# The fifth key tiles of two attention heads as one tile, with mask rows, and the last queries' part added on VectorE

## The reference

```python
scores = scale * np.matmul(q, k.transpose(0, 1, 3, 2))
mask = block_i >= block_j                 # blocks of 64
scores = np.where(mask, scores, -1000000000.0)
scores = scores - np.max(scores, axis=-1, keepdims=True)
attn = np.exp(scores)
attn = attn / (np.sum(attn, axis=-1, keepdims=True) + 1e-09)
return np.matmul(attn, v).astype(np.float32)
```

## Time and profile before

| | |
|---|---|
| median of 3 runs | 1044.92 us (1044.06 to 1045.32) |
| profiled execution | 1045.19 us, its span 1043.0 us |
| mean granted TensorE clock | 0.991 |
| PE busy | 1014.5 us, 97% |
| PE weight loads busy | 933.6 us, 90% |
| POOL busy | 533.9 us, 51% |
| VectorE busy | 443.0 us, 42% |
| ScalarE busy | 368.3 us, 35% |
| DMA, mean | 120 GB/s |

### The profile page before, as it was taken

The page is one execution under the profiler, slowest core; times in us unless marked ns, Lnnn a source line. Parts: engine busy times, 40 slices in busy tenths (PEclk is TensorE's granted clock), DMA queues, the critical chain, the costliest instruction groups (busy, mean ns, idle before and its releaser), DMA issues.

```text
span 1043.0 us, 16716 instructions
## 1 busy us (share of the span) xinstructions
PE 1014.5 (97%) x5927; PEld 933.6 (90%) x5928; DVE 443.0 (42%) x935; ACT 368.3 (35%) x681; POOL 533.9 (51%) x424
## 2 busy tenths in 40 slices
PE   6999999898999999999999999999999999999996
PEld 5899999787989898989899998889898989899895
DVE  6788888674224233332425652222232223222221
ACT  5999988843212222222224413212121212111110
POOL 8689999530000202020202136968778887878752
PEclk9999999999999999999999999999999999999998
DMA  8787886292970101010301166262717163634303
GB/s 174 165 199 193 208 209 169 73 282 75 367 298 2 61 0 61 0 61 0 127 15 62 52 222 177 79 180 69 193 32 217 23 191 70 191 71 141 41 8 45
DMA packets 73682, 125.27 MB, mean 120 GB/s; under 512 B 13073, under 2 KB 30609, under 8 KB 73634
## 3 DMA queue, kind: packets, MB, share of 16 engines
q1 hardware_dynamic: 64594, 103.74, 33.8%
q0 software_dynamic: 8960, 20.61, 9.9%
q10 hardware_dynamic: 80, 0.29, 0.1%
HBM read 78.73 MB, written 36.67 MB: 111 GB/s over the span
## 4 chain that ended last, share of the span: by engine, by line
PE 74%; DVE 1%; ACT 0%; POOLq 0%; issue 0%; DVEq 0%
PE ps_turn L1639 13%; PE ps_x L1615 10%; PE ps_b L1615 10%; PE ps_a L1686 10%; PE ps_x L1704 9%; PE ps_b L1686 9%; PE ps_small L1639 8%; PE ps_a L1595 2%; PE ps_small L1587 1%; PE ps_turn L1577 1%; PE ps_small L1569 0%; POOLq L894 0%; PE ps_small L1570 0%; DVE y_tile L1380 0%; DVE w_raw L1545 0%
## 5 line engine op out<-in xcount | busy, mean ns | idle before, releaser
L1142 POOL DMA_INDIRECT expert_rows<-x_rows,slot_idx x36 | 41.7, 1158 | 307.6 <-DVE slot_idx L1515 298.5
L1199 POOL DMA_INDIRECT out<-y_tile,out_rows x40 | 63.3, 1581 | 76.1 <-DVE y_tile L1380 71.5
L1242 ACT CAST xT_high<-ps_a 128x512 fp32r<-128x512 f32 x40 | 23.3, 587 | 190.3 <-PE ps_a L1595 190.3
L1317 ACT COPY prod<-ps_a 128x384 f32<-128x384 f32 x48 | 23.0, 480 | 163.7 <-PE ps_b L1686 163.7
L1522 DVE TENSOR_TENSOR prod<-ps_b,prod 128x384 f32<-128x384 f32 x48 | 26.8, 557 | 125.5 <-ACT prod L1317 125.5
L1615 PE MATMUL ps_b<-xT_high,w_high 128*128 128x256 f32 (+3 forms) x256 | 77.5, 303 | 0.0
L1639 PE MATMUL ps_turn<-wo_high,hT_high 128*128 128x512 f32 x192 | 76.2, 397 | 1.2 <-DVE hT_low L1371 1.2
L1615 PE MATMUL ps_x<-xT_high,w_high 128*128 128x256 f32 (+3 forms) x256 | 76.9, 300 | 0.0
L1615 PE MATMUL ps_x<-xT_low,w_high 128*128 128x256 f32 (+3 forms) x256 | 76.8, 300 | 0.0
L1615 PE MATMUL ps_x<-xT_high,w_low 128*128 128x256 f32 (+3 forms) x256 | 76.8, 300 | 0.0
L1615 PE MATMUL ps_b<-xT_high,w_low 128*128 128x256 f32 (+3 forms) x256 | 76.8, 300 | 0.0
(11 more groups left out here) (271 smaller groups left out, 3011.7 us busy)
## 6 DMA issues: line engine op xcount, KB each, us to landing
spare<-e_w SPq DMA_DIRECT2D x16, 1024.0 KB, 5.3
w_raw<-e_w SPq DMA_DIRECT2D x16, 1024.0 KB, 8.8
expert_rows<-zeros SPq DMA_DIRECT2D x8, 1290.0 KB, 15.3
ex_rows<-expert_rows SPq DMA_DIRECT2D x40, 258.0 KB, 4.1
k_raw<-kT SPq DMA_DIRECT2D x31, 288.0 KB, 4.9
out<-zeros SPq DMA_DIRECT2D x11, 512.0 KB, 10.3
q_raw<-qT SPq DMA_DIRECT2D x16, 288.0 KB, 4.5
q_mix<-q_top SPq DMA_DIRECT2D x16, 288.0 KB, 3.8
```

The lines of the kernel that those rows point to most:

```text
L1142: nc.gpsimd.indirect_dma_start(out=rows_dram, out_offset=bass.IndirectOffsetOnAxis(ap=slot_idx[:, k, t:t + 1], axis=0), in_=x_rows[:, t, : ...
L1199: nc.gpsimd.indirect_dma_start(out=out, out_offset=bass.IndirectOffsetOnAxis(ap=out_rows[:, j:j + 1], axis=0), in_=y_tile[j][:], in_offset ...
L1242: nc.scalar.copy(xT_high[:, :, j * P:(j + 1) * P], ps_xT[j % XS][:].rearrange("p (c t) -> p c t", t=P)).then_inc(xhigh, 1)
L1317: nc.scalar.copy(prod[f % 2][:], ps_a[f % 2][:, 0:G]).then_inc(a_copied, 1)
```

## The change

The keys of both heads are put in one row of 1152: 576 of head 0, then the last 64 of head 1 (its keys are rolled by 64 on the host), then the first 512 of head 1. Columns 512 to 640 are then the fifth tiles of both heads, 64 keys each. They are one key tile for the last 64 queries of both heads, 128 in all. The cross terms (keys of one head, queries of the other) get -1e9 by two more mask rows. The zero padding of the keys goes, with its memsets.

The fifth tile moves from the units "early0" and "early1" to the unit "first", which now has 384 columns in place of 256, while the early units have 448 in place of 512. Its scores are two matmuls of 128 columns in place of four of 64, its values three of 128 in place of six of 64. v's fifth tile holds head 0's last 64 keys on partitions 0 to 63 and head 1's on 64 to 127, with ones in the other half; it is loaded by two DMAs in place of one, and cast (ACT) and subtracted (POOL) by an instruction of its own. Its output goes to its own 128 columns of heads_out, last_out, and DVE adds it to the outputs taken out, with two instructions behind its take_out and a wait between; out_whole counts them, and the gathering of sums and PE's next "first" values wait for it. ACT copies the last queries' maxima before the exps of "late1" in place of after them, and PE's "first" scores wait for both copies.

```diff
-        k_again = [sb(f"k_again{u}", [P, 2, PADDED], F32R) for u in range(OPERANDS)]
+        k_again = [sb(f"k_again{u}", [P, 2, S], F32R) for u in range(OPERANDS)]
+        last_out = heads_out[:, 512 + P:512 + P + 2 * BLOCK]
...
+        def keys_of(h, begin, end):
+            at = h * (S + BLOCK)
+            return slice(at + begin, at + end)
...
             def load_v(n):
...
                 sp.dma_start(flat[:, 0:FULL], v[n, 0:FULL * P].rearrange("(c p) e -> p c e", p=P)).then_inc(v_loaded, 16)
-                sp.dma_start(flat[0:S - FULL * P, FULL], v[n, FULL * P:S]).then_inc(v_loaded, 16)
+                for h in range(2):
+                    own = slice(h * D, (h + 1) * D)
+                    sp.dma_start(v_raw[own, FULL, h], v[n, FULL * P:S, own]).then_inc(v_loaded, 16)
...
             def gather_sums(n):
+                sp.wait_ge(out_whole, 2 * (n + 1))
                 for h in range(2):
-                    sp.wait_ge(out_taken[h], n + 1)
...
             def low_v(n):
...
                 for h in range(2):
                     part = slice(h * D, (h + 1) * D)
-                    nc.gpsimd.tensor_tensor(v_low[u][:, :, h, part], v_raw[:, :, h], v_high[u][:, :, h, part].bitcast(F32),
+                    nc.gpsimd.tensor_tensor(v_low[u][:, 0:FULL, h, part], v_raw[:, 0:FULL, h], v_high[u][:, 0:FULL, h, part].bitcast(F32),
                                             ALU.subtract).then_inc(v_low_ready, 1)
+                nc.gpsimd.tensor_tensor(v_low[u][:, FULL, 0], v_raw[:, FULL].rearrange("p h e -> p (h e)"), v_high[u][:, FULL, 0].bitcast(F32),
+                                        ALU.subtract).then_inc(v_low_ready, 1)
...
                 nc.vector.tensor_scalar(tmp[n % SLOTS][1], whole_out[1], guard[:, 1:2], None, ALU.add).then_inc(out_taken[1], 1)
+                dve.wait_ge(out_taken[1], n + 1)
+                for h in range(2):
+                    ours = tmp[n % SLOTS][h][:, LAST_AT[h]:LAST_AT[h] + BLOCK]
+                    nc.vector.tensor_tensor(ours, last_out[:, h * BLOCK:(h + 1) * BLOCK], ours, ALU.add).then_inc(out_whole, 1)
...
-                nc.scalar.copy(parts, v_raw[:]).then_inc(v_high_ready, 1)
+                nc.scalar.copy(parts, v_raw[:, 0:FULL]).then_inc(v_high_ready, 1)
+                nc.scalar.copy(v_high[u][:, FULL, 0], v_raw[:, FULL].rearrange("p h e -> p (h e)")).then_inc(v_high_ready, 1)
...
                 each(copy_max, p + 1, 0)
+                each(copy_max, p + 1, 1)
                 each(exps, p, "late1")
-                each(copy_max, p + 1, 1)
...
-                    pe.wait_ge(max_copied, 2 * n + 1)
-                    tiles = [(work[:, SHARED, h * P:(h + 1) * P], h, 0, 0, P) for h in range(2)]
+                    pe.wait_ge(max_copied, 2 * n + 2)
+                    tiles = [(work[:, SHARED, h * P:(h + 1) * P], h, keys_of(h, 0, P), slice(0, P)) for h in range(2)]
+                    tiles += [(work[:, SHARED, 2 * P:2 * P + 2 * BLOCK], slice(0, 2), slice(FULL * P, FULL * P + P), slice(S - BLOCK, S))]
...
-                    tiles = {"early": [(out[:, 0:LATER], h, 0, P, S), (out[:, LATER:LATER + BLOCK], h, 4, S - BLOCK, S)],
+                    tiles = {"early": [(out[:, 0:LATER], h, keys_of(h, 0, P), slice(P, S))],
...
+                    if n:
+                        pe.wait_ge(out_whole, 2 * n)
...
+                    for k, (vs, ps) in enumerate(parts):
+                        mm = nc.tensor.matmul(last_out, vs[:, FULL, 0], ps[:, AT_LAST:COLUMNS], start=k == 0, stop=k == 2)
...
-                        nc.tensor.matmul(later_out[h], vs[:, 0, h], ps[:, h, at:at + LATER], start=k == 0, stop=False)
-                        mm = nc.tensor.matmul(later_out[h][:, LATER - BLOCK:LATER], vs[:, 4, h], ps[:, h, at + LATER:at + LATER + BLOCK],
-                                              start=False, stop=False)
+                        mm = nc.tensor.matmul(later_out[h], vs[:, 0, h], ps[:, at:at + LATER], start=k == 0, stop=False)
...
     for h in range(2):
-        rows_k[masked + h:masked + 2 * full:2, h, 0:S] = 1
-    rows_k[-1, :, 0:S] = 1
+        rows_q[masked + h, h, full * P:S] = 1
+        rows_k[masked + h, 1 - h, full * P:S] = -1e9
+        rows_k[heads + h:heads + 2 * full:2, h] = 1
+    rows_k[-1] = 1
+    rows_k[:, 1] = np.roll(rows_k[:, 1], block, axis=-1)
+    kT = by_pair(k, 4, 2, 3).reshape(pairs, D, 2, S)
+    kT[:, :, 1] = np.roll(kT[:, :, 1], block, axis=-1)
```

More of the change, by code:

```diff
@@ L33, in attention @@
     UNITS = ("first", "early0", "early1", "second0", "second1", "late0", "late1")
-    AT = {"early": 0, "second": LATER + BLOCK, "late": 2 * LATER + BLOCK}
-    WIDE = {"early": LATER + BLOCK, "second": LATER, "late": (LATER - P) + (LATER - 2 * P)}
-    AT_FIRST = sum(WIDE.values())
-    COLUMNS = AT_FIRST + P
+    AT = {"early": 0, "second": LATER, "late": 2 * LATER}
+    WIDE = {"early": LATER, "second": LATER, "late": (LATER - P) + (LATER - 2 * P)}
+    HEAD = sum(WIDE.values())
+    AT_FIRST, AT_LAST = 2 * HEAD, 2 * HEAD + 2 * P
+    COLUMNS = AT_LAST + 2 * BLOCK
     BANK = {"early0": 0, "early1": 1, "second0": 2, "second1": 0, "late0": 1, "late1": 2}
@@ L46, in attention @@
     OUT_AT = (BLOCK, 2 * 512 - P)
+    LAST_AT = (LATER - BLOCK, S - BLOCK)
     tmp, inv_rows, sums, inverses, stored = kept
-    out_taken, sums_in, inv_ready, inv_stored, inv_spread, normalized = done
+    out_taken, sums_in, out_whole, inv_ready, inv_stored, inv_spread, normalized = done
     def after(n, unit):
@@ L253, in _ @@
             nc.gpsimd.memset(neg_max[:], 0.0).then_inc(pads_zeroed, 1)
[L254 to L256 removed]
+            pool.wait_ge(pads_zeroed, 1)
             def rest_q(n):
@@ L435, in _ @@
             act.wait_ge(first_k, 16)
-            nc.scalar.copy(k_again[0][0:D, :, 0:S], k_raw[0][0:D]).then_inc(first_k_again, 1)
+            nc.scalar.copy(k_again[0][0:D], k_raw[0][0:D]).then_inc(first_k_again, 1)
             cast_k(0)
@@ L476, in scores @@
                     pe.wait_ge(max_found, at + {"two1": 1, "three0": 2, "three1": 3, "four": 5}[part])
-                top, again = q_top[u][0:MAX_ROW], k_again[u][0:MAX_ROW]
+                top, again = q_top[u][0:MAX_ROW], in_a_row(k_again[u])[0:MAX_ROW]
                 if part == "one":
                     for h in range(2):
-                        mm = nc.tensor.matmul(work[:, SHARED + 1, 2 * P * h:2 * P * (h + 1)], top[:, h, P:2 * P], again[:, h, 0:2 * P],
+                        mm = nc.tensor.matmul(work[:, SHARED + 1, 2 * P * h:2 * P * (h + 1)], top[:, h, P:2 * P], again[:, keys_of(h, 0, 2 * P)],
                                               start=True, stop=True)
@@ L521, in turned_scores @@
                     h, out = int(unit[-1]), work[:, BANK[unit]]
-                    tiles = {"early": [(out[:, 0:LATER], h, 0, P, S), (out[:, LATER:LATER + BLOCK], h, 4, S - BLOCK, S)],
-                             "second": [(out[:, 0:LATER], h, 1, P, S)],
-                             "late": [(out[:, 0:LATER - P], h, 2, 2 * P, S), (out[:, LATER - P:2 * LATER - 3 * P], h, 3, 3 * P, S)]}[unit[:-1]]
-                for out, h, c, begin, end in tiles:
-                    keys = slice(c * P, (c + 1) * P)
-                    nc.tensor.matmul(out, k_parts[u][:, h, keys], q_mix[u][:, h, begin:end], start=True, stop=False)
-                    mm = nc.tensor.matmul(out, k_again[u][:, h, keys], q_top[u][:, h, begin:end], start=False, stop=True)
+                    tiles = {"early": [(out[:, 0:LATER], h, keys_of(h, 0, P), slice(P, S))],
+                             "second": [(out[:, 0:LATER], h, keys_of(h, P, 2 * P), slice(P, S))],
+                             "late": [(out[:, 0:LATER - P], h, keys_of(h, 2 * P, 3 * P), slice(2 * P, S)),
+                                      (out[:, LATER - P:2 * LATER - 3 * P], h, keys_of(h, 3 * P, 4 * P), slice(3 * P, S))]}[unit[:-1]]
+                for out, h, keys, queries in tiles:
+                    nc.tensor.matmul(out, in_a_row(k_parts[u])[:, keys], q_mix[u][:, h, queries], start=True, stop=False)
+                    mm = nc.tensor.matmul(out, in_a_row(k_again[u])[:, keys], q_top[u][:, h, queries], start=False, stop=True)
                 mm.then_inc(turned_done, 1)
@@ L564, in idle @@
                 for _ in range(count):
-                    nc.tensor.matmul(heads_out[:, 0:512], pT_high[:, 0, 0:P], pT_high[:, 0, 0:512], start=True, stop=True)
+                    nc.tensor.matmul(heads_out[:, 0:512], pT_high[:, 0:P], pT_high[:, 0:512], start=True, stop=True)
             def each(do, n, what):
```

96 lines of the change are left out of this document (44 added, 52 removed).

## The result

The changed kernel takes 1051.73 us (median of 4 runs, 1051.01 to 1052.92), before takes 1045.01 beside it: a ratio of 1.0057, with a 95% interval of 1.0036 to 1.0078. It is 4 to 8 us slower. The profiled execution took 1051.76, with a span of 1049.9 (before 1043.0).

What follows compares the result with a forecast made beforehand. A loop through SP and POOL was taken to hold PE in later pairs. Loop and k_again +3.1, last pairs -1.3 and the end +0.55 made +2.35 on 1045.19: 1047.54, as a median 1047.2; range 1043.5 to 1050.0.

Steps and rivals of the forecast that it cites:

- a holding loop: PE's scores "one": 11.8 to 12.0 us apart from about pair 5, idle time before each, would show the forecast right.
- DVE, the step that failed: DVE's two adds and their wait: 0.55 us per pair, covered by 1.6 idle per pair, so no cost until the end.
- The width of "first": ACT's exps and lows: same elements in sum, twice 64 fewer and once 128 more; no cost counted.
- ACT: zero: ACT's extra high_v instruction, some 0.2 us, and later arrivals: covered by 1.25 idle per pair; 0.2 to 0.7 if not.
- Rival (c): DVE becomes the bound, deciding from about 1.7 us more per pair; 1051 us; chance 0.06.
- The loop: low_v, SP's DMA list, spread of inverses, POOL's work, next low_v: holds PE in later pairs, 11.53 rising to 11.90 per pair.
- Its third DMA: SP's extra load of v: adds 0.56 us to SP's part of the loop, which goes round once in two pairs.
- PE's own work: Ten 64-column matmuls go, five of 128 come, 0.11 us each: -0.55 per pair, PE alone needing 10.72.
- low_v's price: POOL's low_v as three instructions instead of two: 0.17 us more per pair, between 0 and 0.45.
- The end: After the last pair nothing covers DVE's adds and wait, since PE idles for DVE there: +0.55 us.
- The clock: TensorE's clock might fall as PE idles about 1.2 us in each pair; nothing was counted for it.
- the chances of the same and of slower: Whole-time outcome: same 0.43, slower 0.49, faster or slower meaning below 1042.8 or above 1047.0 us.

Runs made afterwards that it cites:

- adds gone: The changed kernel without DVE's two adds and their wait, the last queries' fifth-tile part left out of the output: 1049.22 us, ratio 1.0045.
- adds later: The changed kernel with DVE's two adds of the previous pair moved behind the max of "two0", same work: 1047.78 us, ratio 1.0032.
- the fifth tile as a unit of its own: Changed kernel, adds behind max of "two0", v packed into one DMA, "first" 256 wide, 128-column unit "last" behind "second1": 1045.07 us, ratio 1.0006.
- blocks of PE moved besides: The fifth tile as a unit of its own, both early units' turned scores before "two0", turned scores "last" behind "four": 1045.61 us, ratio 0.9998.
- the fastest one: The fifth tile as a unit of its own, with its three values matmuls moved behind values "late1" on PE: 1043.03 us, ratio 0.9983.

## Why the prediction was wrong

The forecast was 1047.2 with a range to 1050.0; 1051.7 lies outside. The sign was right for the wrong reason, and so was the spacing of "one": 11.8 to 12.0 was named as the sign of a holding loop, 11.8 came, and without the idle time that should stand before each.

- **DVE, the step that failed.** "DVE idles 2.84 of 20 us, 1.6 per pair: covered." The idle time was that of the whole pair; what counted was the row from the max of "one" to that of "three1", which had none, and 0.38 to "four". I forecast 0.55 for the adds and their wait; they took 0.39, so the price was no worse than thought, and it lay on the path. Without them the pair is 0.40 shorter; with them elsewhere in the row, 0.3.
- **The width of "first", same failure.** "The elements of exps and lows are the same in sum." In sum, yes, but they moved to a place for which PE waits. Alone in the kernel before this costs 0.35 per pair, on ACT and DVE together. "ACT: zero" is thereby in doubt: ACT's own share is not shown.
- **Rival (c)** named the right engine. Its point of decision, 1.7 us more, came from the same average; by the row it was 0.38.
- **The loop.** Forecast 11.90 per pair, measured 11.87 (ends of low_v from 67.73 to 174.58, nine pairs). That agreement shows little, since PE's own pace is 11.81; a better one is the two pairs held by the loop with the adds gone, 11.92 and 11.97. PE never met it: with 11.81 of its own it kept 2.4 us of distance to k_again at 164.88. Where the pair is shorter (adds gone, adds later) it shows in the last pairs. Its third DMA was mis-sized: 0.43 per pair in the kernel before, not 0.28, and 4.9 us in all. That it is paid once per issue is not shown, since packing v in the kernel before gave nothing back.
- **PE's own work.** 64 columns behind a 448 cost 0.08, not 0.11: values "early0" went from 0.85 (128.68 to 129.53) to 0.61 (146.65 to 147.26) for three fewer. The five of 128 cost 0.11 each as forecast. Summed over the blocks PE's work falls by about 0.33, not 0.55, and 0.24 of what was added lies in the part that PE leads.
- **POOL.** The 2.27, 2.01 and 2.00 that I read as low_v's price were delayed ones. In the kernel before the first four took 1.69 to 1.71, and of the later ones all but the last 2.0 to 2.3; after, all sixteen took 1.83 to 1.86. Like for like that is 0.14 more, near the 0.17 forecast, and the delays are gone. Harmless here.
- **The end.** Forecast +0.55, measured 0.40 (idle 3.64 instead of 3.24).
- **The clock.** "I count nothing" holds for the pairs (1.00 from 31 us to the end of attention) but not for the start: a dip of some 7 us, of which unused matmuls won back 0.4 net.
- **A slip in the sums.** By their own parts the chances of the same and of slower are 0.44 and 0.48, not 0.43 and 0.49. Nothing hangs on it.

The sum by what was measured, between the starts of "one": the first is 0.24 later (9.70 instead of 9.46), the next 0.18 more, pair 0 takes 14.28 instead of 13.33 (+0.95, the dip in it), the 13 after it 153.51 instead of 147.23 (+6.28: 13 x 0.54, less 0.7 that before loses to its loop), and from the last "one" to the first matmul behind attention 25.35 instead of 24.79 (+0.56). That is 8.21 (213.81 instead of 205.60). The span grew by only 6.9. Most of the 1.3 between is the clock right behind attention, in code that the change doesn't touch (first before, then after; columns as in the earlier trace rows):

```profile
204.00:212.00 8.00, 6.40 (x16) 5.08 (x17) 6.56 (x12) 6.89 (x13) 3.48 (x6) 0.57 0.76 203
```
```profile
214.00:218.00 4.00, 4.00 (x12) 3.10 (x12) 3.82 (x8) 4.00 (x8) 1.77 (x4) 0.57 0.74 216
```

The stretch at 0.50 lasts about 6.8 us before and 3.4 after, and the first sixteen matmuls of that stage take 6.43 (205.60 to 212.03) and 5.32 (213.81 to 219.13): 1.11 of the 1.3. Attention alone thus lost more than the whole kernel shows. Both lengths occur in the profiles of the other kernels (3.3 us with the fifth tile as a unit of its own, 6.8 with blocks of PE moved besides), so this looks like chance in the execution; no run was made for it.

## What to carry to other kernels

An engine's idle share over a stage is no cover for an instruction: follow the row in which that instruction stands, from the event that starts it to the one that another engine waits for, and count only the gap at its end. Cut a period by who leads each part; work added in a part that the other engine leads is nearly free, and the same work moved across the border costs in full. An instruction made wider counts where it stands, even if as many elements go elsewhere. And before a time per period is read as the price of a change, look at the granted clock of that stretch: a longer wait can bring it down and make the price look larger than it is.

## What the runs showed of the hardware

Two VectorE instructions of 128x256 with all operands in SBUF took 1.73 and 2.76 us together, while a single one of 128x256 with an operand in PSUM took 0.42; GpSimd was at work beside them (k_parts from 98.36 to 101.33 beside the pair of 98.85 to 101.61). Near the end of attention, inside an idle stretch of GpSimd of 5.61 us, the same two took 0.75:

```profile
237.11 0.75 DVE L344 TENSOR_TENSOR junk<-junk 128x256 f32<-128x256 f32 x2
```

The cast of q (64x1152, also SBUF to SBUF) varies in the same way, 0.74 at 150.84 in the kernel after, 1.38 at 109.53 in the fastest one. The Trainium skill (SBUF — State Buffer, section SBUF: two separate sides) says that GpSimd and some VectorE operations lock each other out of a shared port; these rows fit that, and no run separates the port from another cause tied to GpSimd's work.

One further DMA issue in SP's row cost the kernel before 4.9 us, though it carries no new bytes, and dropping one gave nothing. PE in the start-up of the kernel after idled 0.97 and 0.83 us (ahead of 20.67 and of 22.39) and was granted 0.50 of its clock for some 7 us; with unused matmuls in the first gap it kept 1.00, and so did the kernel before with idles of 1.10 and 0.56. With two long instructions in DVE's row PE idled about 1.8 in each pair, and the clock fell in some pairs and not in others.
